# Attention, mixture of experts and an ELU layer in one kernel: projections and head product one tile step later, ELU in PSUM, gate scaling on ScalarE

## The reference

```
attention, batch 2, 8 heads, 768 tokens, head size 64, proj 64 x 6
  q_bits, k_bits = (q @ proj > 0), (k @ proj > 0);  a query sees only keys with the same 6 bits
  out = softmax(where(same bits, q k^T / 8, -1e9)) @ v        -> x: 1536 x 512
experts, 8 of them, 512 -> 1024 -> 512
  expert = argmax(x @ w_gate);  x = gate * (relu(x @ w1[expert]) @ w2[expert])
last layer, 512 -> 2048 -> 512
  h = x @ w_in;  g = where(h > 0, h, exp(min(h, 0)) - 1);  y = g @ w_out
```

## Time and profile before

| | |
|---|---|
| median of 3 runs | 899.59 us (899.03 to 900.49) |
| the profiled execution | 900.39 us, span of its instructions 898.7 us |
| PE busy | 793.3 us, 88% of the span |
| DVE, ACT, POOL busy | 48%, 39%, 42% |
| attention, experts, last layer | to 307, to 584 and from 588 us of the span |

### The profile page before, as it was taken

The page is one execution under the profiler, slowest core; times in us unless marked ns, Lnnn a source line. Parts: engine busy times, 40 slices in busy tenths (PEclk is TensorE's granted clock), DMA queues, the critical chain, the costliest instruction groups (busy, mean ns, idle before and its releaser), DMA issues.

```text
span 898.7 us, 14057 instructions
## 1 busy us (share of the span) xinstructions
PE 793.3 (88%) x4070; PEld 668.3 (74%) x4071; DVE 428.0 (48%) x705; ACT 353.5 (39%) x707; POOL 380.6 (42%) x462
## 2 busy tenths in 40 slices
PE   3899899989999509999999999916999999999998
PEld 2788888888888407888887778705777877778886
DVE  2888887888788601122212221165433444344333
ACT  1776767777777302121222122201233433233332
POOL 1433433344344179599999999077000000000000
PEclk9999999999999858999999999957999999999999
DMA  6565374344433055466566656132000000001001
GB/s 165 126 197 151 101 196 132 80 128 114 120 103 85 25 184 186 133 197 200 188 195 201 208 180 200 43 118 82 12 12 23 11 37 1 0 0 47 1 1 47
DMA packets 71214, 95.06 MB, mean 106 GB/s; under 512 B 32144, under 2 KB 34192, under 8 KB 71184
## 3 DMA queue, kind: packets, MB, share of 16 engines
q1 hardware_dynamic: 63792, 78.44, 30.0%
q10 hardware_dynamic: 5472, 9.96, 3.4%
q0 software_dynamic: 1920, 6.29, 2.1%
HBM read 59.54 MB, written 16.25 MB: 84 GB/s over the span
## 4 chain that ended last, share of the span: by engine, by line
PE 50%; issue 16%; DVE 10%; POOL 9%; DMA 6%; ACT 6%; SPq 1%; POOLq 1%; DVEq 1%; ACTq 0%
PE ps_s L630 8%; PE ps_s L632 8%; PE ps_s L631 8%; PE ps_t L729 5%; PE ps_t L731 5%; PE ps_t L730 5%; POOL w_lo L486 4%; DVE stats L936 4%; DMA late_stage<-in_moe_w_dram 3%; PE ps_p L546 2%; ACT probs L796 2%; DVE pt_lo L949 2%; POOL w_hi L482 2%; PE ps_t L580 2%; DVE yg L1091 1%
## 5 line engine op out<-in xcount | busy, mean ns | idle before, releaser
L796 ACT ACTIVATE probs<-ps_s,stats 128x768 f32<-128x768 f32 x96 | 95.6, 995 | 34.0 <-POOL stats L436 32.3
L936 DVE TENSOR_REDUCE stats<-ps_s 128x1 f32<-128x768 f32 x96 | 91.7, 955 | 28.8 <-PE ps_s L564 27.7
L949 DVE TENSOR_TENSOR pt_lo<-ps_t,pt_hi 128x384 fp32r<-128x384 f32 x192 | 97.1, 548 | 10.6 <-ACT pt_hi L789 10.3
L789 ACT ACTIVATE pt_hi<-ps_t 128x384 fp32r<-128x384 f32 x192 | 84.3, 496 | 43.1 <-PE ps_t L580 43.1
L434 POOL TENSOR_SCALAR stats<-stats 128x1 f32<-128x1 f32 x96 | 21.1, 220 | 164.5 <-DVE stats L936 164.4
L486 POOL TENSOR_TENSOR w_lo<-stage,w_hi 128x1024 fp32r<-128x1024 f32 x36 | 86.0, 2388 | 0.0
L486 POOL TENSOR_TENSOR w_lo<-late_stage,w_hi 128x1024 fp32r<-128x1024 f32 x36 | 85.6, 2388 | 0.0
L630 PE MATMUL ps_s<-w_hi,gT_hi 128*128 128x512 f32 x192 | 77.6, 404 | 6.4 <-DVE gT_lo L1121 6.4
L580 PE MATMUL ps_t<-ident,probs 128*128 128x128 f32 x576 | 79.7, 274 | 0.8 <-DVE pt_lo L949 0.5
L729 PE MATMUL ps_t<-yT_hi,w_hi 128*128 (+1 forms) x192 | 77.8, 405 | 1.5 <-DVE yT_lo L1095 1.4
L731 PE MATMUL ps_t<-yT_hi,w_lo 128*128 (+1 forms) x192 | 76.7, 400 | 0.0
(11 more groups left out here) (147 smaller groups left out, 1685.4 us busy)
## 6 DMA issues: line engine op xcount, KB each, us to landing
stage<-in_moe_w_dram SPq DMA_DIRECT2D x72, 256.0 KB, 3.0
...
```

What stands on the lines that cost most here:

```text
L789: a(pt_hi[gb][:, half * HALF:(half + 1) * HALF, uu * P:(uu + 1) * P], ps_t[:, half, 0:HW].rearrange("p (t c) -> p t c", c=P), ACT.Copy).th ...
L796: a(probs[:, s % 4].rearrange("p (h c) -> p h c", h=2), ps_s[:, 2 * (s % 2):2 * (s % 2) + 2, 0:HW], ACT.Exp, bias=stats[:, 2, c], scale=st ...
L936: v_.tensor_reduce(stats[:, 0, c], ps_s[:, 2 * (s % 2):2 * (s % 2) + 2, 0:HW], AX.XY, ALU.max).then_inc(max_found, 1)
L949: v_.tensor_tensor(pt_lo[gb][where], ps_t[:, half, 0:HW].rearrange("p (t c) -> p t c", c=P), pt_hi[gb][where].bitcast(F32), ALU.subtract). ...
```

## The change

It has two independent parts. In attention the first projection moves from the end of u = 1 to u = 2, the second from u = 2 to u = 3, both right after the scores, and `finish_head` with `move_rows` from the end of u = 4 to the end of u = 5. In the last layer relu and the two SBUF tiles `elu_r`, `elu_g` go: DVE writes max(exp - 1, h) back over h in PSUM, hi and lo are made from there, and inner(f + 2) waits until the lo part of step f is made. Gate scaling moves from DVE to ACT, and the moves of the next block's transposed tiles come one f later.

```diff
+        FINISH_AT = 5
@@ PE, attention
-                    if u == 2 and has_next(i, j):
-                        pe.wait_ge(prep_moved, chunks_before(h) + 3)
-                        project(1 - j, 1, ps_p)
+                    if u in (2, 3) and has_next(i, j):
+                        pe.wait_ge(prep_moved, chunks_before(h) + u)
+                        project(1 - j, u - 2, ps_p)
...
-                    if u == 1 and has_next(i, j):
-                        pe.wait_ge(prep_moved, chunks_before(h) + 2)
-                        project(1 - j, 0, ps_p)
-                    if u == 4 and has_last(i, j):
+                    if u == FINISH_AT and has_last(i, j):
                         pe.wait_ge(prep_moved, chunks_before(h) + (4 if has_next(i, j) else 0))
                         finish_head(h - 1)
@@ PE, inner
-                pe.wait_ge(h_low, m + 1)
-                pe.wait_ge(h_high, m + 1)
+                pe.wait_ge(g_lo, m + 1)
@@ ACT, last layer
+            def scale_yg(t, q, turn):
+                act.wait_ge(yg_in[q], turn)
+                a(yg[:, q], yg[:, q], ACT.Copy, scale=gate[:, ds(t, 1)]).then_inc(yg_scaled, 1)
...
-                    act.wait_ge(h_made, m + 1)
-                    act.wait_ge(g_made, m + 1)
-                    act.wait_ge(h_low, m + 2 + 1)
-                    a(elu_r[:], ps_t[:, f % 2], ACT.Relu).then_inc(h_high, 1)
+                    act.wait_ge(h_low, m + 1)
                     a(elu_e[:], elu_e[:], ACT.Exp).then_inc(h_exp, 1)
...
-                    a(gT_hi[:, f % 2], elu_g[:], ACT.Copy).then_inc(g_hi, 1)
-                    if f in TURN_AT and not last:
-                        turn_move(blk + 1, (blk + 1) % 2, TURN_AT.index(f))
+                    a(gT_hi[:, f % 2], ps_t[:, f % 2], ACT.Copy).then_inc(g_hi, 1)
+                    if f - 1 in TURN_AT and not last:
+                        turn_move(blk + 1, (blk + 1) % 2, TURN_AT.index(f - 1))
+                    if f + 1 in TURN_AT and not last:
+                        q = TURN_AT.index(f + 1)
+                        scale_yg((blk + 1) * BT + q, q, (blk + 1) * 16 + 16)
@@ DVE, last layer
-            def scale_yg(t, q, turn):
-                dve.wait_ge(yg_in[q], turn)
-                v_.tensor_scalar(yg[:, q], yg[:, q], gate[:, ds(t, 1)], None, ALU.mult).then_inc(yg_scaled, 1)
...
-                    v_.scalar_tensor_tensor(elu_g[:], elu_e[:], -1.0, elu_r[:], ALU.add, ALU.add).then_inc(g_made, 1)
+                    v_.scalar_tensor_tensor(ps_t[:, f % 2], elu_e[:], -1.0, ps_t[:, f % 2], ALU.add, ALU.max).then_inc(g_made, 1)
                     dve.wait_ge(g_hi, m + 1)
-                    v_.tensor_tensor(gT_lo[:, f % 2], elu_g[:], gT_hi[:, f % 2].bitcast(F32), ALU.subtract).then_inc(g_lo, 1)
+                    v_.tensor_tensor(gT_lo[:, f % 2], ps_t[:, f % 2], gT_hi[:, f % 2].bitcast(F32), ALU.subtract).then_inc(g_lo, 1)
```

More of the change, by code:

```diff
@@ L232, in attention_moe_mlp @@
         yg_scaled, yT_made, yT_hi_moved, yT_lo_moved = sem("yg_scaled"), sem("yT_made"), sem("yT_hi_moved"), sem("yT_lo_moved")
-        h_made, h_low, h_exp, h_high = sem("h_made"), sem("h_low"), sem("h_exp"), sem("h_high")
+        h_made, h_low, h_exp = sem("h_made"), sem("h_low"), sem("h_exp")
         g_made, g_hi, g_lo, g_used = sem("g_made"), sem("g_hi"), sem("g_lo"), sem("g_used")
@@ L267, in slots_of @@
         def slots_of(i):
-            return range(5 if isinstance(i, int) and i == PAIRS else SPP)
+            return range(FINISH_AT + 1 if isinstance(i, int) and i == PAIRS else SPP)
         def has_next(i, j):
@@ L734, in outer @@
             def outer(blk, f):
-                pe.wait_ge(g_lo, blk * NF + f + 2)
+                pe.wait_ge(g_lo, blk * NF + f + 3)
                 for q in range(BT):
@@ L877, in layer @@
                     m = blk * NF + f
-                    act.wait_ge(h_made, m + 1)
+                    act.wait_ge(h_low, m + 1)
+                    a(elu_e[:], elu_e[:], ACT.Exp).then_inc(h_exp, 1)
                     act.wait_ge(g_made, m + 1)
-                    act.wait_ge(h_low, m + 2 + 1)
-                    a(elu_r[:], ps_t[:, f % 2], ACT.Relu).then_inc(h_high, 1)
-                    a(elu_e[:], elu_e[:], ACT.Exp).then_inc(h_exp, 1)
-                    act.wait_ge(g_made, m + 2)
                     if f != 1:
                         act.wait_ge(g_used, blk * (NF - 1) + max(f - 1, 0) + 2)
-                    a(gT_hi[:, f % 2], elu_g[:], ACT.Copy).then_inc(g_hi, 1)
-                    if f in TURN_AT and not last:
-                        turn_move(blk + 1, (blk + 1) % 2, TURN_AT.index(f))
+                    a(gT_hi[:, f % 2], ps_t[:, f % 2], ACT.Copy).then_inc(g_hi, 1)
[4 more added lines that the diff above has]
+                        scale_yg((blk + 1) * BT + q, q, (blk + 1) * 16 + 16)
+            for q in range(BT):
+                scale_yg(q, q, 16)
             for q in range(BT):
@@ L938, in body @@
                         move_qk(1 - j, h + 1, u, ps_p)
-                    if u == 2 and has_next(i, j):
-                        move_bits(1 - j, h + 1, 1, ps_p)
-                    if u == 3 and has_last(i, j):
+                    if u in (2, 3) and has_next(i, j):
+                        move_bits(1 - j, h + 1, u - 2, ps_p)
+                    if u == 4 and has_last(i, j):
                         dve.wait_ge(guarded, h)
@@ L950, in body @@
                                              pt_hi[gb][where].bitcast(F32), ALU.subtract).then_inc(lo_moved, 1)
-                    if u == 1 and has_next(i, j):
-                        move_bits(1 - j, h + 1, 0, ps_p)
-                    if u == 4 and has_last(i, j):
+                    if u == FINISH_AT and has_last(i, j):
                         move_rows(i, h - 1)
@@ L1110, in layer @@
                     m = blk * NF + f
-                    if f + 1 in TURN_AT and not last:
-                        q = TURN_AT.index(f + 1)
-                        scale_yg((blk + 1) * BT + q, q, (blk + 1) * 16 + 16)
                     dve.wait_ge(h_made, m + 1)
-                    dve.wait_ge(g_lo, m + 1)
                     v_.tensor_scalar(elu_e[:], ps_t[:, f % 2], 0.0, None, ALU.min).then_inc(h_low, 1)
                     dve.wait_ge(h_exp, m + 1)
-                    dve.wait_ge(h_high, m + 2 + 1)
-                    v_.scalar_tensor_tensor(elu_g[:], elu_e[:], -1.0, elu_r[:], ALU.add, ALU.add).then_inc(g_made, 1)
+                    v_.scalar_tensor_tensor(ps_t[:, f % 2], elu_e[:], -1.0, ps_t[:, f % 2], ALU.add, ALU.max).then_inc(g_made, 1)
                     dve.wait_ge(g_hi, m + 1)
-                    v_.tensor_tensor(gT_lo[:, f % 2], elu_g[:], gT_hi[:, f % 2].bitcast(F32), ALU.subtract).then_inc(g_lo, 1)
-                    if f in TURN_AT and not last:
-                        turn_move(blk + 1, (blk + 1) % 2, TURN_AT.index(f))
-            dve.sem_inc(g_made, 1)
-            dve.sem_inc(g_lo, 1)
-            dve.sem_inc(h_low, 2)
-            dve.sem_inc(h_high, 2)
+                    v_.tensor_tensor(gT_lo[:, f % 2], ps_t[:, f % 2], gT_hi[:, f % 2].bitcast(F32), ALU.subtract).then_inc(g_lo, 1)
+                    if f - 1 in TURN_AT and not last:
+                        turn_move(blk + 1, (blk + 1) % 2, TURN_AT.index(f - 1))
+            dve.sem_inc(g_lo, 2)
             dve.sem_inc(g_used, 2)
@@ L1133, in _ @@
             dve.sem_inc(out_stored, 16)
-            for q in range(BT):
-                scale_yg(q, q, 16)
             for q in range(BT):
```

2 lines of the change are left out of this document (removed).

## The result

| | before | after |
|---|---|---|
| median of the runs made side by side, us | 900.04 (899.03 to 900.6, 4 runs) | 870.54 (869.61 to 871.24, 4 runs) |
| ratio, 95% interval | | 0.9671 [0.9657, 0.9686] |
| profiled execution and its span, us | 900.39, 898.7 | 870.19, 868.5 |

What follows compares the result with a forecast made beforehand. PE was taken as the bound, with idle time in attention and at the last layer's start. Gains of 8.65, 7.63 and 7.6 sum to 23.9 us, giving 875.5 us, with a range of 863 to 886.

Steps and rivals of the forecast that it cites:

- the forecast's own case (870 to 880): Whole kernel: the forecast's sum roughly holds and the time lands in 870 to 880 us; chance 0.55.
- Last layer, first 8.65: Last layer's start: with gate scaling on ACT, inner(0) starts 8.65 us earlier after the gathers.
- Second, 7.63: Last layer, inner(0) to the end of outer(0): 7.63 us gained, 5.4 idle and 2.1 clock.
- The new wait: Last layer, before inner(2): PE newly waits 1.06 us for the first ELU's lo part.
- Attention 7.6: Attention: 0.45 us net in each of 14 heads, some 1.3 in head 0, none in head 15; 7.6 us.
- The 2.2 removed: Attention: PE's old waits at both projections and the head product go, together 2.2 us a head.
- The three terms given back: Attention, new waits a head: 0.95 at `turn_qk(0)`, 0.7 at step 5's transposes, 0.1 at the first projection.
- the forecast's own sign of being wrong (under 16.8): Attention: the forecast is wrong if a head takes under 16.8 or over 17.9 us; 17.4 expected.
- The rival with the waits falling together (15 to 20): Attention: waits given back coincide, gaining 15 to 20 us, for a time of 863 to 869; chance 0.13.
- nothing that DVE or ACT saves there can be seen: Last layer from 631.99 on: PE is the bound, busy 263.37 of 263.61 us, so no gain there.
- Costed at nothing: Rest of last layer: later moves and inner(f + 2)'s ELU wait cost 0; uncovered, about 1 us at each of two block borders.
- The rule that spoke against the edit: Last layer's ELU: three PSUM reads per f might be slow; at twice 0.69 for add and subtraction, gain 6.2.

Runs made afterwards that it cites:

- moves_at_f: The kernel after, with the moves of the next block's turned tiles back in step f; 896.75 us, ratio 0.997.
- elu_sbuf_out: The kernel after, with the ELU add writing to SBUF and hi and lo made from there; 877.08 us, ratio 0.9754.

## Why the prediction held, and where its sizes were off

The mechanisms were right in kind and place, and the forecast's own case (870 to 880) holds the result, though by only 0.5 us. The sum was 6.3 us short, most of it in one term, attention. By its steps:

- **Last layer, first 8.65: 8.65.** The order behind the gathers did what was said. That the number is exact is in part luck. The scaling on ACT takes 0.72, not the 0.62 taken from a row without a per-partition scale, and from the fourth gather to inner(0) it is 589.87 - 580.62 = 9.25, 0.3 more than the sum had. But the fourth gather itself came 0.3 sooner after the last expert matmul (7.99, before 8.27).
- **Second, 7.63: 8.27.** The new wait was put at 1.06. inner(1)'s last matmul starts at 596.81 and the next could start 0.23 later, at 597.04; it starts at 598.01, so 0.97. The add at 0.69, read off the min, came out at 0.70. The full clock through outer(0), which runs from 600.92 to 603.71, held (1.00 in 600:604, against 0.54 in the earlier trace rows). The 0.64 more came from the clock: it rose 3.2 us after inner(0)'s start (0.96 in 593:594), so inner(0) and inner(1) took 7.17 (589.87 to 597.04), while the forecast carried over the 7.80 of before.
- **Attention 7.6: 11.2, the largest miss.** The 2.2 removed is confirmed: in the longer head PE's own work is 17.05 less the two waits, 0.87 + 0.58, so 15.60, where the forecast had 15.6. In the shorter one (16.91) the wait at `turn_qk(0)` is 0.73 instead of 0.87 and the rest is the same. The three terms given back were each too large: 0.95 measured 0.87 and 0.73, 0.7 measured 0.58, 0.1 measured 0. Net 0.78 a head on the means of 17.76 and 16.98, not 0.45; over 14 heads that is 4.6 more. What is then left for head 0 and the rest is 0.3 where 1.3 was put. Each term was good to about 0.2; the error is that of a small difference of larger numbers, times 14. It brought the heads near the forecast's own sign of being wrong (under 16.8). The rival with the waits falling together (15 to 20) is refuted: both waits stand side by side in 12 heads.
- **Rest of the last layer, 0: 1.95.** The step "nothing that DVE or ACT saves there can be seen" failed by a little. Of the kernel before, PE and ACT:

```profile
643.40 0.40 PE L632 MATMUL ps_s<-w_lo,gT_hi 128*128 128x512 f32 x1
643.81 0.46 PE L729 MATMUL ps_t<-yT_hi,w_hi 128*128 x1
```

```profile
643.07 0.60 ACT L881 ACTIVATE elu_r<-ps_t 128x512 f32<-128x512 f32 x1 [1.44 <-DVE elu_e L1116]
```

PE starts the product 0.41 after the matmul before instead of 0.23, without a bracket, because relu (643.07 + 0.60) had to read the bank first; relu waited for DVE's min, and that stood behind the tile's move (641.66 + 0.69). It does so at 8 turned tiles, 0.18 each: 1.4 of the 1.95. With relu gone, so is this.

- **Costed at nothing.** The moves one f later were, with a cover of about 1 us. That is confirmed for the kernel after; what `moves_at_f` shows is that the cover exists only there. The forecast priced its loss at 1 us at each of two block borders; it is 2.1 at 8 tiles, with a fallen clock on top, 25.6 us in all. So this was the costliest term to get wrong, and the forecast had it right.
- **The rule that spoke against the edit.** Three PSUM reads per f instead of one cost nothing: 0.69, 0.70, 0.69. The Trainium skill, VectorE: DVE Perf Modes, section Rules for kernel authors, offers copying to SBUF for many operations; here, an ELU kept in SBUF behind the add cost 6.5 us (`elu_sbuf_out`), because the subtraction was held while GpSimd was busy (7.87). The trace agrees with the other alternative of that rule, to accept the PSUM source.
- **The held instructions.** The Trainium skill, SBUF — State Buffer, section SBUF: two separate sides, says that VectorE wants the shared ports for two SBUF inputs or for its two-port mode. By that rule the add with one PSUM input is free; the trace agrees, 0.69 against 7.87 for two SBUF inputs at the same time of the run. The scaling is held with one SBUF input (7.27); free it takes 0.48 to 0.52, less than the add's 0.69. That fits the two-port mode, which no row here names.
